# One store of 288 KB per step in place of two of 144 KB, in the gate stage of a fused attention and two-MLP kernel

## What is computed

```python
kv  = einsum('bhsd,bhse->bhde', k, v)          # attention without softmax, 8 batches, 8 heads, 576 rows, 64 columns
out = einsum('bhsd,bhde->bhse', q, kv)
x   = out / sqrt(mean(out*out, -1) + 1e-6) * g_norm   # -> [4608, 512]
h   = sigmoid(x @ w_gate) * (x @ w_val)        # 512 -> 1536
y   = h @ w_out                                # 1536 -> 512
g   = clamped square: 0 below -1, itself above 1, (t+1)^2/4 between, of t = y @ w_in   # 512 -> 2048
o   = g @ w_out2                               # 2048 -> 512
```

## Time and profile before

| | |
|---|---|
| median of three runs | 1707.41 us (1705.03 to 1708.48) |
| profiled execution, its own time | 1706.1 us |
| its span | 1704.3 us |
| mean granted clock of TensorE | 0.991 of 2.4 GHz |
| TensorE busy | 1658.4 us (97%) |
| VectorE busy | 1216.3 us (71%) |
| ScalarE busy | 886.0 us (52%) |
| POOL busy | 202.2 us (12%) |
| stores of h | 192 of 144 KB |

### The profile page before, as it was taken

How to read it: one execution, slowest core, us unless ns; L and a number is a source line. 1 busy time by engine, 2 the same in 40 slices (tenths; PEclk the granted TensorE clock), 3 DMA queues, 4 the chain that set the end, 5 groups by cost and what they waited for, 6 DMA issues and landing times. The chain is left out here.

```text
span 1704.3 us, 31798 instructions
## 1 busy us (share of the span) xinstructions
PE 1658.4 (97%) x12475; PEld 1627.3 (95%) x12475; DVE 1216.3 (71%) x1725; ACT 886.0 (52%) x1612; POOL 202.2 (12%) x266
## 2 busy tenths in 40 slices
PE   8999999999999999999999999999997899999999
PEld 6789999999999998999999999999997799999999
DVE  3677777777777775877778787777775577777664
ACT  4666666655555554544445555555553444444442
POOL 3410000015242221200002500000002100000000
PEclk9999999999999999999999999999998999999999
DMA  7444444334777777744334333333439844444451
GB/s 256 153 136 140 146 140 140 111 128 133 245 242 239 240 264 238 242 154 153 116 136 164 133 133 132 140 121 122 162 134 318 276 124 125 143 138 140 124 124 38
DMA packets 229317, 278.91 MB, mean 164 GB/s; under 512 B 33072, under 2 KB 172848, under 8 KB 229168
## 3 DMA queue, kind: packets, MB, share of 16 engines
q1 hardware_dynamic: 217104, 233.35, 41.4%
q0 software_dynamic: 12064, 43.52, 7.8%
HBM read 156.76 MB, written 120.06 MB: 162 GB/s over the span
## 5 line engine op out<-in xcount | busy, mean ns | idle before, releaser
L1542 PE MATMUL x<-t_hi,v_lo 128*128 128x288 f32 x1664 | 498.6, 300 | 19.0 <-ACT c_kept L1009 11.5
L1543 PE MATMUL x<-t_lo,v_hi 128*128 128x288 f32 x1664 | 493.7, 297 | 0.0
L1544 PE MATMUL x<-t_hi,v_hi 128*128 128x288 f32 x1664 | 492.3, 296 | 0.0
L1542 PEld LDWEIGHTS x<-t_hi,v_lo 128*128 128x128 f32 x1664 | 314.2, 189 | 24.3 <-ACT c_kept L1009 12.2
L1544 PEld LDWEIGHTS x<-t_hi,v_hi 128*128 128x128 f32 x1664 | 315.3, 190 | 0.0
L1543 PEld LDWEIGHTS x<-t_lo,v_hi 128*128 128x128 f32 x1664 | 314.5, 189 | 0.1
L1542 PE MATMUL y<-t_hi,v_lo 128*128 128x288 f32 x832 | 250.2, 301 | 5.7 <-DVE c L1087 1.7
L1543 PE MATMUL y<-t_lo,v_hi 128*128 128x288 f32 x832 | 247.0, 297 | 0.0
L1544 PE MATMUL y<-t_hi,v_hi 128*128 128x288 f32 x832 | 246.5, 296 | 0.0
L1542 PE MATMUL x<-v_hi,t_lo 128*128 128x256 f32 x576 | 164.0, 285 | 5.2 <-DMA v_lo<-fold_lo 2.8
L1542 PEld LDWEIGHTS y<-t_hi,v_lo 128*128 128x128 f32 x832 | 157.5, 189 | 10.4 <-DVE c_tile L1087 3.7
(11 more groups left out here) (187 smaller groups left out, 3520.8 us busy)
## 6 DMA issues: line engine op xcount, KB each, us to landing
g_scratch<-c_tile SPq DMA_DIRECT2D x128, 288.0 KB, 2.4
gq<-g_scratch SPq DMA_DIRECT2D x64, 512.0 KB, 6.1
h_scratch<-gate SPq DMA_DIRECT2D x192, 144.0 KB, 1.8
hq<-h_scratch SPq DMA_DIRECT2D x32, 864.0 KB, 5.1
stage<-w_in POOLq DMA_DIRECT2D x68, 256.0 KB, 3.3
kv_ring<-kv_in SPq DMA_DIRECT2D x30, 512.0 KB, 4.5
fold_hi<-fold_hi SPq DMA_DIRECT2D x14, 896.0 KB, 6.0
fold_lo<-stage SPq DMA_DIRECT2D x14, 896.0 KB, 4.9
```

What stands on the lines that cost most here:

```text
L1542: nc.tensor.matmul(dst, s_lo, m_hi, start=start, stop=False, skip_group_check=True)
L1543: nc.tensor.matmul(dst, s_hi, m_lo, start=False, stop=False, skip_group_check=True)
L1544: return nc.tensor.matmul(dst, s_hi, m_hi, start=False, stop=stop, skip_group_check=True)
```

## The change

The two stores of a step become one of 288 KB, issued where the second half's was, behind `h_ready` (and `h0_ready`). The semaphores `h0_stored` and `h1_stored` become one pair `h_stored`. Both additions into the tile (L1353, L1362) now wait for the store of the whole tile. In DRAM the two halves of a row lie side by side, so a row's run is 2304 bytes in place of twice 1152.

```diff
-        h0_stored = [sem(f"h0_stored{i}") for i in range(2)]
-        h1_stored = [sem(f"h1_stored{i}") for i in range(2)]
+        h_stored = [sem(f"h_stored{i}") for i in range(2)]
...
-            def h_place(k, half):
+            def store_h(k):
                 b, s = divmod(k, A_SETS)
                 row, n = (s, b) if b < B else (A_SETS + s, b - B)
-                return h_dram[row, :, S * n + C * half:S * n + C * (half + 1)]
-
-            def store_h0(k):
                 sp.wait_ge(h0_ready, k + 1)
-                sp.dma_start(h_place(k, 0), gate[:, k % 2, 0, :]).then_inc(h0_stored[k % 2], 16)
-
-            def store_h1(k):
                 sp.wait_ge(h_ready, k + 1)
-                sp.dma_start(h_place(k, 1), gate[:, k % 2, 1, :]).then_inc(h1_stored[k % 2], 16)
+                sp.dma_start(h_dram[row, :, S * n:S * (n + 1)], flat(gate[:, k % 2, :, :])).then_inc(h_stored[k % 2], 16)
...
-                if k:
-                    store_h0(k - 1)
                 if k in FOLDS:
                     store_fold_hi(FOLD1_TASK + FOLDS[k])
...
                 if k:
-                    store_h1(k - 1)
+                    store_h(k - 1)
...
                 if k == A_STEPS - 8:
-                    all_stored(sp, h0_stored, k, 16)
-                    all_stored(sp, h1_stored, k, 16)
+                    all_stored(sp, h_stored, k, 16)
                     load_quarter_h(0)
...
-                    reach(dve, h1_stored[(k - 1) % 2], 16 * ((k - 1) // 2))
+                    reach(dve, h_stored[(k - 1) % 2], 16 * ((k - 1) // 2))
                     add(gate[:, (k - 1) % 2, 1, :], Y[(k - 1) % 2][:, 0:C], kept[:, 1 + (k - 1) % 2, :]).then_inc(c12_ready, 1)
...
-                    reach(dve, h0_stored[k % 2], 16 * (k // 2))
+                    reach(dve, h_stored[k % 2], 16 * (k // 2))
                     add(gate[:, k % 2, 0, :], Z[0][:, 0:C], kept[:, 0, :]).then_inc(c11_ready, 1)
```

More of the change, by code:

```diff
@@ L497, in _ @@
                     load_quarter_h(2)
-            all_stored(sp, h0_stored, A_STEPS, 16)
-            all_stored(sp, h1_stored, A_STEPS, 16)
+            all_stored(sp, h_stored, A_STEPS, 16)
             def store_y(b, m):
@@ L1400, in _ @@
                             if b == 0:
-                                all_stored(dve, h0_stored, A_STEPS, 16)
-                                all_stored(dve, h1_stored, A_STEPS, 16)
+                                all_stored(dve, h_stored, A_STEPS, 16)
                             reach(dve, y_stored[m], 32 * b)
```

## The result

| | before | after |
|---|---|---|
| median (nine runs each, same chip) | 1705.42 us (1703.17 to 1712.83) | 1711.05 us (1708.83 to 1716.32) |
| profiled execution, its own time | 1706.1 us | 1713.53 us |
| its span | 1704.3 us | 1711.7 us |
| mean granted clock of TensorE | 0.991 | 0.992 |

A forecast was written before the change was run, and what follows sets the result against it. TensorE, busy for 97% of the span, was taken as the bound. Adding 2.1 us (steps 86 to 89) and 1.0 us (steps 90 to 93) to 1707.4 gave 1710.5 us, range 1706.5 to 1714.8.

The forecast's parts named there:

- the ordinary stretch: Gate stage from 500 to 540 us: as a sign of being right, it still holds 302 matmuls.
- c(88): Addition into gate tile's first half (L1362), bracket giving the step; predicted waiting until 640.5, pause 4.4 us, net +2.1 us.
- 96 of 192 issues: All gate steps: the removed store issues, 0.32 us of SP each, were worth nothing because SP idles anyway.
- The same single fall: After the longer pause in steps 86 to 89: TensorE's clock falls once as before, costing the same 1.5 us.
- Steps 90 to 93: End of the gate stage: step 92's addition waits 3.0 us for a store beside POOL's loads, net +1.0 us.
- inside the free 2.1 us: Step 93's addition, due at 668.8: loads ending by 669.5 to 671 delay it only within TensorE's 2.1 us margin.
- Two waits that SP passes earlier: SP's wait for the first half ahead of the fold and key/value issues goes; claimed cost: nothing.
- A wait stays inside the 2.1 us: Gate steps whose store landed with under 0.6 us to spare: additions late by under 2.1 us don't stop TensorE.
- steps 54 and 60: Mid-stage stores beside an x load and two fold stores miss the deadline: cost taken as 0, up to 0.5 us each.
- Rival 1: Loads and stores take turns: step 90's store lands in about 4.8 us, only +2.1 us remain, 1709.5; chance 0.12.
- Rival 2: It hides or gains: fold stores and POOL's loads end sooner near the stage's end, 1704 to 1707.5 us; chance 0.20.
- Rival 3: Late additions delay the next stores in steps 90 to 92: +5 to +10 us, 1712.5 to 1717.5; chance 0.22.

The follow-up runs named there:

- e6: Changed kernel plus 20 matmuls, whose result nothing reads, in TensorE's pause ahead of product 6 of step 89: 1709.88 us, ratio 1.0015 to before.
- e9: Changed kernel where SP again waits for the first half (h0_ready) ahead of each high fold store: 1711.10 us in five runs, ratio 1.0042 to before.
- e3: Changed kernel with its waits kept, but two stores of 144 KB issued behind them in place of one: 1714.08 us, ratio 1.0049 to before.
- e1: Changed kernel with whole-tile stores up to step 83 and stores by halves from step 84: 1711.18 us, ratio 1.0030 to before.
- e4: Changed kernel with the high fold store of iteration 87 issued behind the store of step 86, not ahead: 1709.84 us, ratio 1.0022 to before.
- e5: Changed kernel with POOL's second pair of folded weight loads held until product 3 of step 88: 1710.58 us, ratio 1.0017 to before.
- e11: Changed kernel (whole stores) with POOL's first two pairs of weight loads issued early, near 566 and 600 us: 1709.08 us, ratio 1.0038 to before.
- e8: Changed kernel where VectorE does the second multiplication ahead of the next step's addition into the first half: 1732.44 us, ratio 1.0145 to before.
- e12: The kernel of e11 with the SP wait of e9 added ahead of each high fold store: 1710.26 us, ratio 1.0032 to before.
- e2: Changed kernel with stores by halves up to step 83 and whole-tile stores from step 84: 1711.12 us, ratio 1.0029 to before.
- e7: Kernel before (stores by halves) with POOL's second pair of weight loads held until product 3 of step 88: 1707.24 us, ratio 1.0003 to before.
- e10: Kernel before (stores by halves) with POOL's first two pairs of weight loads issued early, near 566 and 600 us: 1701.96 us, ratio 0.9979 to before.

## Why the prediction was right in sign and too small

The measured median, 1711.05 us, lies 0.5 us above the forecast and inside its range. That it is so near is luck: the difference to before is 5.8 us for 3.1, and the runs of before came out 2 us lower this time. Within 0.2% and slower by more had nearly the same chance; it came out on the slower side, 0.8 us beyond the 2.5 to 5 us that the forecast gave itself. Of its signs, the ordinary stretch held, and c(88) did but for the 1.66 us that c(87) was late. VectorE's waits for stores of h grew to 21.1 us and not to 13, the stage ended 7.7 us later and not 3, and two of the signs of being wrong showed: a small new pause ahead of 620 us, at 368.88, and more than 0.5 us of movement there.

- **"96 of 192 issues ... worth nothing; an ordinary step: nothing is waited for."** Right: 302 matmuls, and an ordinary store landed in 2.1 to 2.2 us for 2.4 assumed.
- **c(88) and the pause.** The mechanism was right. Predicted: c(88) at 640.5, pause of 4.4 us to 641.5. Measured: c(88) at 642.65 with c(87) 1.66 us late already, so 640.99 by itself, and a pause of 5.24 us to 643.64. The release was 0.5 us later than predicted. The store of step 87 landed in 2.1 us, ahead of c(89), which did not wait, as predicted.
- **"The same single fall, at the same 1.5 us."** One fall, but a longer one: the clock is at 0.50 from 641.5 to 648.3 us. The 21 matmuls from 643.64 to 648.65 took 5.0 us where 21 x 0.132 = 2.8 would do: 2.2 us. This term was 0.7 us too small by the matmuls themselves, though e6 won back only 1.6 us of it. I also read the earlier trace rows wrongly: "6 matmuls in place of 7.5" counts those that overlap a microsecond. In order of time they start 0.24 us apart, which is 4.2 per us.
- **Steps 90 to 93: +1.0 us.** From c(91) to c(95) the difference grows from 4.88 to 6.28, by 1.4 us. The amount is near, the place isn't: c(92) waited 2.33 us (3.0 predicted) and caused no pause; c(93), called "inside the free 2.1 us", waited 3.57 us and caused the pause of 1.06 us at 675.15. The store behind it, issued at 668.1, took 5.9 us, beside the pair of loads issued near 665. So these terms give 3.1 + 0.5 + 0.7 + 0.4 = 4.7 us for the 4.6 us of the end. (By its own numbers c(92) was due at 660.37 + 2.1 = 662.5, not 662.3; that is 0.2 us.)
- **"Two waits that SP passes earlier ...: nothing."** This step failed, and cost 1.9 us in the trace. The load of x took 7.7 us for 5.8, so all behind it in the queue lands late: the store of step 84, issued at 618.9, took 5.4 us and c(86) waited 2.09 us; fold_lo landed so late that ScalarE's cast ran at 626.77 with a wait of 1.05 us, where before it ran at 625.12 without one. VectorE's work on that task started 1.66 us later, and c(87) stands behind it. e9 gives the wait back with one line, and the load's delay and the 1.9 us are gone; how the wait acts on the load stays open. In e3, which lacks the wait too, the load landed in 6.1 us and 1.3 us were lost between the same points all the same, in small waits at other steps: the load isn't the only way to lose there.
- **"A wait stays inside the 2.1 us."** Only in part. c(56) waited 1.79 us and 0.2 us remained; c(62) waited 1.99 us and 0.5 us remained; c(41) waited 0.97 us and 0.6 us remained. I had taken 0 and up to 0.5 us as a bound for steps 54 and 60. c(41) stands behind the store of step 39, one of the four that had landed with under 0.6 us to spare (0.33 for the 144 KB) and that I had dismissed with this sentence. The 2.1 us are the margin of product 6 alone. Behind c(41) VectorE has the splits for the next block, and TensorE stood 0.46 us for `t_lo`, not for ScalarE's copy. The sum of the middle is 1.0 to 1.2 us in the traces of after, e1, e3, e4, e5, e6, e9 and e11 (2.0 in e8, 2.5 in e12), which store whole tiles there, and at most 0.2 us in e2, e7 and e10, which store halves. In e9 and e12 a fall of the clock to 0.50 for 3.4 us, from 494.7 and 494.0 us, is in the sum; c(k) falls back by 1.0 and 1.25 us there, so that e9 would have 0.15 us without it.
- **The rivals.** Rival 1 (turns between the queues) asked for 4.8 us at step 90; it took 6.6, and 7.5 in e4 for the store of step 86 with nothing of its queue ahead. The Trainium skill, "DMA: Bandwidth & Descriptors", section "Queues, rings and completion order", says that a DMA engine takes turns between its queues packet by packet. The packets of the changed kernel's trace agree with that only once the store of step 90 has begun to move. From its issue at 660.5 to 664.5 us, then from 664.5 to 667.1 us, POOL's queue (q0) and SP's (q1): packets, MB, share of the engines:

```profile
q0 software_dynamic: 199, 1.12, 96.6%
q1 hardware_dynamic: 1, 0.00, 0.2%
...
q0 software_dynamic: 115, 0.61, 69.5%
q1 hardware_dynamic: 143, 0.29, 31.0%
```

So the store waited about 4 us for its first packet, and then took its turns in 2.6 us. In e4 the store of step 86 waited 4 us as well: SP's queue moved no packet from 633.2 to 637.2 us. Why the first packet comes so late beside the loads, no run here shows. Rival 2 fails: fold_hi and the store behind it landed no earlier. Rival 3 (the loop) fits c(92) and c(93), two late ones in a row, and e8's shorter waits, but it doesn't run away: c(94) waits for no store, and e8's end is no shorter.

**What stays open.** What makes the last load of x land late: it took 5.5 to 6.1 us in before, e2, e3, e7, e9 and e10, and 7.7 to 8.2 us in after, e1, e4, e5, e6 and e8 (8.6 in e11 and 6.6 in e12, where POOL's loads had moved). The distance of fold_hi doesn't sort them: it is 1.84 us in e3 and 2.29 in e8. And why e9's total didn't fall: its trace ends stage A 5.9 us late counted from c(40), 1.8 us less than the change, while its five runs say the opposite within their interval.

## What to carry to other kernels

A merged transfer inherits the earliest deadline and the latest producer of its parts. So look for its price at the steps where bulk transfers stand in the same queue or beside it, not at the ordinary step, and for each such step at every engine behind the late instruction, not at one margin. A wait in a DMA queue also sets when what follows goes out; when it is taken out, look again at the landings behind it. And where a transfer waits for a crowd, see whether the crowd can move (here the loads for the next stage, 0.2%, with an interval from 0.07 to 0.36%), before the small transfers are changed.

## What the runs showed of the hardware that I had not expected

- The granted clock around a pause: before, a pause of 2.06 us ended at 644.97, and the clock was at 0.50 from 646.2 to 649.6 us. After, it fell inside the pause of 5.24 us that ended at 643.64, and was at 0.50 from 641.5 to 648.3 us; TensorE was at work for 4.7 us of these. In e5 a pause just as long as before's, 2.06 us at 652.64, was followed by no fall (1.00 from 645 to 675 us), nor was one of 2.11 us at 641.76 in e4 (1.00 from 634 to 655 us), while one of 1.75 us at 494.17 in e9 was, and one of 1.75 us at 493.95 in e4 wasn't. The length of the pause alone doesn't decide.
- A transfer of 144 or 288 KB alone in its own queue takes 6.6 to 7.5 us beside 768 KB loads of another queue, against 1.7 and 2.2 us by itself. Of the 6.6 us about 4 passed before its first packet moved.
- Two late stores of 144 KB were not better than one of 288 KB: ratio 1.0049 against 1.0034, with intervals that overlap.
